# Row weights for a transposed output: widened by VectorE and transposed, in place of 16 fp32 passes that spread them

## What is computed

```python
scores = q @ k.T / sqrt(D), masked causally
a = exp(scores - rowmax);  a /= a.sum(-1) + 1e-9
local = a @ v
q_p = phi(q)                       # elu(q) + 1
mem_out = (q_p @ M_prev) / (q_p @ z_prev + 1e-6)
attn = g * mem_out + (1 - g) * local      # g = sigmoid(beta), per head
x = moe(attn);  out = moe2(x)      # h = x @ w_in; activation; @ w_out
```

## Time and profile before

| | |
|---|---|
| profiled execution | 1050.11 us |
| its span | 1048.3 us |
| median of 3 runs | 1049.9 us |
| PE busy | 1015.0 us (97%) |
| DVE busy | 486.9 us (46%) |
| ACT busy | 414.9 us (40%) |
| POOL busy | 274.9 us (26%) |
| L852 (the 16 passes), all pairs | 17.5 us in 256 records |

### The profile page before, as it was taken

The page is one execution under the profiler, slowest core; times in us unless marked ns, Lnnn a source line. Parts: engine busy times, 40 slices in busy tenths (PEclk is TensorE's granted clock), DMA queues, the critical chain, the costliest instruction groups (busy, mean ns, idle before and its releaser), DMA issues.

```text
span 1048.3 us, 16398 instructions
## 1 busy us (share of the span) xinstructions
PE 1015.0 (97%) x6256; PEld 924.5 (88%) x6256; DVE 486.9 (46%) x1063; ACT 414.9 (40%) x935; POOL 274.9 (26%) x276
## 2 busy tenths in 40 slices
PE   5999999999999999999999999999999999999998
PEld 4776676679999999999999999999999999999997
DVE  6777878775634444344444443323323223232222
ACT  4677777763323233232332455222223232232222
POOL 7788888877800000000000366000000000000000
PEclk9999999999999999999999999999999999999999
DMA  5444444412200000000000143000000000000000
GB/s 169 142 133 141 133 131 132 125 58 76 93 14 1 1 1 0 0 0 0 1 1 1 61 123 110 1 1 31 1 30 0 0 30 0 26 5 1 31 1 31
DMA packets 30204, 48.02 MB, mean 46 GB/s; under 512 B 3264, under 2 KB 13504, under 8 KB 30144
## 3 DMA queue, kind: packets, MB, share of 16 engines
q1 hardware_dynamic: 27584, 38.81, 12.2%
q0 software_dynamic: 2560, 8.39, 2.6%
HBM read 42.47 MB, written 4.72 MB: 45 GB/s over the span
## 4 chain that ended last, share of the span: by engine, by line
PE 91%; DVE 4%; ACT 2%; DMA 1%; POOL 1%; issue 0%; SPq 0%; POOLq 0%; DVEq 0%; ACTq 0%
PE ps L910 26%; PE ps L909 25%; PE ps L908 25%; PE ps L875 4%; PE ps L803 3%; PE ps L852 2%; DVE prob L590 2%; PE ps L784 2%; PE ps L863 1%; PE ps L791 1%; DVE probT L633 1%; ACT turned L442 1%; DVE klo L572 1%; PE ps L788 1%; PE ps L845 1%; ACT probT L421 1%
## 5 line engine op out<-in xcount | busy, mean ns | idle before, releaser
L910 PE MATMUL ps<-xparts,W 128*128 128x384 f32 x768 | 257.8, 336 | 0.0
L908 PE MATMUL ps<-xparts,W 128*128 128x384 f32 x768 | 257.7, 335 | 0.0
L909 PE MATMUL ps<-xparts,W 128*128 128x384 f32 x768 | 257.2, 335 | 0.0
L723 DVE TENSOR_TENSOR glo<-act_t,ghi 128x384 fp32r<-128x384 f32 x192 | 110.8, 577 | 220.6 <-ACT ghi L502 220.6
L502 ACT CAST ghi<-act_t 128x384 fp32r<-128x384 f32 x192 | 98.7, 514 | 229.8 <-PE ps L910 210.8
L300 POOL TENSOR_TENSOR W<-stage,W 128x512 fp32r<-128x512 f32 x64 | 83.0, 1307 | 324.7 <-ACT W L544 321.7
L908 PEld LDWEIGHTS ps<-xparts,W 128*128 128x128 f32 x768 | 144.3, 188 | 4.2
L909 PEld LDWEIGHTS ps<-xparts,W 128*128 128x128 f32 x768 | 144.1, 188 | 4.1
L910 PEld LDWEIGHTS ps<-xparts,W 128*128 128x128 f32 x768 | 144.1, 188 | 0.0
L908 PE MATMUL ps<-ghi,W 128*128 128x384 f32 x384 | 128.3, 334 | 0.0
L909 PE MATMUL ps<-glo,W 128*128 128x384 f32 x384 | 128.3, 334 | 0.0
(11 more groups left out here) (109 smaller groups left out, 1384.0 us busy)
## 6 DMA issues: line engine op xcount, KB each, us to landing
qraw<-in_qT SPq DMA_DIRECT2D x16, 320.0 KB, 3.2
vn<-in_vN SPq DMA_DIRECT2D x16, 320.0 KB, 2.9
kraw<-in_kT SPq DMA_DIRECT2D x16, 288.0 KB, 3.2
qn<-in_qN SPq DMA_DIRECT2D x16, 288.0 KB, 2.8
zb<-in_zN SPq DMA_DIRECT2D x32, 144.0 KB, 3.1
out_x<-ostage SPq DMA_DIRECT2D x18, 256.0 KB, 2.0
stage<-in_moe_w_in POOLq DMA_DIRECT2D x16, 256.0 KB, 3.6
stage<-in_moe_w_out POOLq DMA_DIRECT2D x16, 256.0 KB, 3.3
```

What stands on the lines that cost most here:

```text
L723: nc.vector.tensor_tensor(glo[:, f % SLOTS, :], a, ghi[:, f % SLOTS, :].bitcast(F32), ALU.subtract).then_inc(glo_done, 1)
L908: nc.tensor.matmul(dst, w_lo_, x_hi_, start=first, stop=False)
L909: nc.tensor.matmul(dst, w_hi_, x_lo_, start=False, stop=False)
L910: return nc.tensor.matmul(dst, w_hi_, x_hi_, start=False, stop=last)
```

## The change

The row weights are first written 64 times side by side by VectorE (`widen`, a new tile `rwide` of 128 x 8 x 64), and `turn_row` transposes the four 128 x 128 blocks of that tile. `widen` stands between maximum(p + 1, 3) and low_k(p + 2) in VectorE's order; it waits for `row_step` (1/den written), and `turn_row` waits for `row_wide`.

```diff
+        rwide = sb("rwide", [P, 2 * FULL, D], where=att)
...
+            def widen(p):
+                dve.wait_ge(row_step, 4 * p + 2)
+                nc.vector.tensor_copy(rwide[:], rw[:, 0, 0:2 * FULL].unsqueeze(2)
+                                      .broadcast_to([P, 2 * FULL, D])).then_inc(row_wide, 1)
...
                 if more:
                     maximum(p + 1, 3)
+                widen(p)
                 if more2:
                     low_k(p + 2)
...
             def turn_row(p):
                 room(p, T_ROW)
+                pe.wait_ge(row_wide, p + 1)
                 for m in range(FULL):
-                    for e in range(2):
-                        last = nc.tensor.matmul(ring(T_ROW)[e * D:(e + 1) * D, m * P:(m + 1) * P],
-                                                rw[:, 0, 2 * m + e:2 * m + e + 1].broadcast_to([P, D]), ident[:],
-                                                start=True, stop=True)
+                    last = nc.tensor.transpose(ring(T_ROW)[:, m * P:(m + 1) * P], rwide[:, 2 * m:2 * m + 2, :],
+                                               ident[:])
                 last.then_inc(t_full, 1)
```

More of the change, by code:

```diff
@@ L150, in build @@
         phi_part, phi_sum, phi_norm = sem("phi_part"), sem("phi_sum"), sem("phi_norm")
-        norm_step, row_step = sem("norm_step"), sem("row_step")
+        norm_step, row_step, row_wide = sem("norm_step"), sem("row_step"), sem("row_wide")
         weighed, v_done = sem("weighed"), sem("v_done")
```

## The result

The changed kernel takes 1083.9 us (median of 4 runs, 1082.12 to 1084.31) against 1049.96 us: a ratio of 1.0321, 95% interval 1.0308 to 1.0334, so 3.2% slower. The profiled execution took 1082.12 us with a span of 1080.3.

A forecast was written before the change was run, and what follows sets the result against it. VectorE's stretch ahead of L788 was taken to bound each attention pair. 13 x 1.40 = 18.2, pair 0 0.79, pair 14 -0.18, pair 15 -0.49: +18.3 on 1050.11, 1068.4, as median 1068.2 us; range 1060 to 1086.

The forecast's parts named there:

- rival (c): TensorE's clock falls in its emptier wait: 1085 us with falls in every second pair, 1076 if half as long; chance 0.25.
- what TensorE is spared: At turn_row, four transposes replace 16 passes: 0.49 us a pair, only 0.18 on the path because memory waits for empty_rest.
- The path: Between 123.4 and 126.1 us VectorE's eviction, klo and maxima set L788, without slack, so delay there lengthens the pair.
- The copy's length: VectorE's 128x512 fp32 SBUF copy, from its start to the next start: 0.35 us taken, between 0.08 and 0.61.
- Who goes first: The copy ahead of klo lets GpSimd's waiting L318 in first, shifting klo and L788 by 1.58 us.
- Rival (b): klo keeps its turn despite waiting L318, so the shift is the copy's length alone: +1.4, 1051.5 us; chance 0.13.
- rival (a): The one-input copy doesn't exclude GpSimd; L318 starts at 124.37, klo shifts 1.32 us whatever L, 1064.8 us; chance 0.13.
- so `memory` could start at 129.27: After turn_row, TensorE's memory starts 0.04 us after ScalarE's empty_rest ends at 129.23, instead of at 129.45.
- Pair 15: Last pair: no exponentials stand between L442 and L436 on ScalarE, so the whole 0.49 us is gained.
- pair 0: First pair: TensorE itself is late, a slack of 0.61 us, leaving 0.79 us of added time.
- What was covered: VectorE's remaining work in the pair stays hidden behind its 1.25 us wait ahead of L645; GpSimd's later steps move less.

The follow-up runs named there:

- The reciprocal: The changed kernel with widen computing 1/den straight into the wide tile by a VectorE reciprocal instead of copying it; 1145.1 us, ratio 1.0907.
- filler run: The changed kernel with 10 more products of 320 columns on TensorE between turn_tail and score(p+1, 4), into PSUM columns nothing reads; 1077.47 us, ratio 1.027.

## Why the prediction was right or wrong

The direction and the range held: 1083.9 us lies in 1060 to 1086. The single value, 1068.2, was 15.7 us too low, because the case that came was rival (c) on top of the forecast, to which I had given 0.25. Against the profiled execution (1082.12 us) the sum of 1068.4 is 13.7 too low: 11.9 are the falls of the clock, 1.7 what TensorE is spared. The other three runs are 1.6 to 2.2 us longer, at a mean granted clock of 0.976 against 0.982, which more or longer falls would explain; they have no trace. That the range held is partly luck: ten falls of the length and price that I took, 2.5 us, would have given 1093, outside it. It held because nine of the ten were half as long.

- *The path.* That VectorE sets L788 between 123.4 and 126.1 us held: moving the copy behind klo and the maxima 4 and 5 took the whole loss away.
- *The copy's length.* Taken as 0.35, measured 0.34 from start to start. The Trainium skill, "VectorE: DVE Perf Modes", section "Mode 2×_2P", with two elements a cycle gave the estimate of 0.33; the row of L639 above agrees, even with an input that repeats each number 64 times.
- *Who goes first.* Held. Shift of L788's place: 1.58 forecast; measured from the copy's start to klo's end it is 142.85 - 140.62 = 2.23, less the 0.67 of klo alone, 1.56. Rival (b) is out by the copy of 8 numbers, rival (a) by the run with klo first. How L319 fares was right as well: it ends 1.35 us after the copy gives way (140.96 to 142.31), as forecast. The Trainium skill, "SBUF — State Buffer", section "Who interferes with whom", has it that whoever issues first holds the pair for the whole instruction and the other blocks. The rows of klo, qlo and the copy of 512 agree, and add what happens when VectorE has two claims in a row. The reciprocal, which kept neither L319 nor L322 out, made no such claim.
- *What TensorE is spared.* This term was mis-sized: 0.18 us a pair, measured 0.02 with the copy out of the way. The step that failed is "so `memory` could start at 129.27", and with it the 0.49. I took the 0.04 us between ScalarE's end and TensorE's next start from L852; at L869 it is 0.15, and L869 itself takes 0.02 to 0.03 longer. Where ScalarE isn't late, the four transposes take 0.59 ahead of `memory` and not the 0.44 that I read ahead of L835, so that at most 0.34 could be had and not 0.49. The period without a fall is 15.56 and not 14.03 + 1.40 = 15.43 for this reason, 13 x 0.13 = 1.7 us of the miss. Pair 15 (-0.3, -0.49 taken) has the sign forecast; pair 0 (0.6, 0.79 taken) has it too, but by what the first `to_x` does from trace to trace that shows nothing.
- *The clock.* The step that failed is the choice of the likeliest. I had worked out that TensorE would be emptier in its new wait than it was ahead of the one fall of the kernel before, and yet put that case at 0.25, on the guess that large products in the stretch would keep the clock up. They didn't. The working itself held: 1.5 of 3.6 us forecast, 1.57 measured (155.90 to 159.50). The price of a long fall was about right: I took 2.5 us for 6.5 us at half clock, by a factor of 1.6 that no row showed. The first of the ten pairs, with 6.8 us at half clock, lost 2.46 us; the nine others, each with about 3.4 us of it, lost 0.94 to 1.19. Worked back, that is a factor of 1.57 in the long fall and of 1.4 to 1.5 in the short ones. With a fall in every second pair (c) had given 1076 to 1085; it was ten of 13, mostly short ones. The filler run shows that the falls were a cost of their own. The prediction's sentence on the Trainium skill, "TensorE: Matmul & The Clock Gate", section "HAM oscillation", is looser than the page: the case there is a kernel whose waits for data are longer than its bursts of products. In the pairs here the wait ahead of L795 is 1.63 us, and the clock fell in ten of 13. So the page didn't make (c) the rule as plainly as the prediction has it, and what decides is the rows.
- *What was covered.* VectorE's and GpSimd's later work stayed hidden, as said: VectorE waits 2.60 us ahead of `to_x` in the pair shown, where it waited 1.25.
- *Slips in the sums.* With L = 0.08, pair 0 is 1.31 - 0.61 - 0.18 = 0.52 and not 0.29. The figures of (a) and (b) are against the profiled execution, 0.2 above the median. Neither moves the range.

## What to carry to other kernels

Where GpSimd and VectorE both work out of SBUF, look for the instruction that is first by a few ns, and ask what a new instruction ahead of it will let in: here 0.07 us of work cost 1.27 us a pair, since the price is the other engine's whole instruction. Then ask whether the wait that this opens on TensorE may cost its clock. Compare the stretch with the emptiest ones that the trace shows beside the granted clock, and where they are as empty as one that preceded a fall, count the fall as likely; it is a warning, not a rule, as the next section shows. And a step that TensorE is spared is worth nothing until the step that is late next, here an eviction of ScalarE, is moved too.

## What the runs showed of the hardware that I had not expected

- A VectorE reciprocal of 128x512 fp32 lasts 3.35 us, 6.5 ns an element, against 0.42 for a copy of the same size; that of 128x9 lasts 0.20.
- The busy share of a stretch doesn't tell by itself whether the clock falls. In the changed kernel TensorE was busy 1.77 of 3.40 us in the following stretch, and the clock stayed at 1.00; in the stretch from 156.40 shown above it was 1.87 of 3.50, and it fell. Taken at the same place of both pairs, up to 143.94 and 159.50, TensorE was busy 1.57 of 3.60 us in each.

```profile
140.80:144.20 3.40, 1.77 (x13) 1.12 (x13) 3.40 (x7) 1.83 (x5) 3.32 (x3) 1.00 0.41 98
```

- Pairs that do the same work in the same order fall or don't: three of 13 escaped in the changed kernel, six of 13 in the run with the copy of 8 numbers. They come in a regular order: pairs 2, 7 and 12 escape in the changed kernel, 1, 5 and 10 with klo first, every second one in the run with the copy of 8. What sets the order was not settled. Runs of such a kernel also differ more, 1070.70 to 1077.27 us there (mean granted clock 0.991 in the shortest, 0.979 to 0.984 in the others), against 1049.11 to 1049.87 for the kernel before beside it.
